# Where the buffers that TensorE reads stand in SBUF: one place in a 2048-byte line instead of two

## The reference

```python
# 1. attention with a state (delta rule): batch 4, 8 heads, 768 steps, head size 48
for t in range(S):
    y[:, :, t] = einsum('bhd,bhde->bhe', q[:, :, t], state)
    v_old = einsum('bhde,bhd->bhe', state, kt)
    state = state + bt * einsum('bhd,bhe->bhde', kt, vt - v_old)
# x = y as 3072 tokens x 384
# 2. eight experts of width 1024; P is a softmax-like gate, balanced in 8 Sinkhorn rounds
out = 0
for e in range(8):
    h = maximum(x @ w1[e], 0)            # 384 -> 1024
    out += P[:, e:e + 1] * (h @ w2[e])   # 1024 -> 384
# 3. one wide layer of width 2048
h = x @ w_in                             # 384 -> 2048
return (h * cos(h)) @ w_out              # 2048 -> 384
```

## Time and profile before

| | |
|---|---|
| median of three executions | 2347.82 us |
| the profiled execution | 2351.72 us |
| its span, first to last instruction | 2350.0 us |
| mean granted TensorE clock | 0.972 of 2.4 GHz |
| TensorE matmul busy | 2256.2 us (96%) |
| VectorE, ScalarE, GpSimd busy | 1012.5, 741.9, 686.6 us |

### The profile page before, as it was taken

The page is one execution under the profiler, slowest core; times in us unless marked ns, Lnnn a source line. Parts: engine busy times, 40 slices in busy tenths (PEclk is TensorE's granted clock), DMA queues, the critical chain, the costliest instruction groups (busy, mean ns, idle before and its releaser), DMA issues.

```text
span 2350.0 us, 40688 instructions
## 1 busy us (share of the span) xinstructions
PE 2256.2 (96%) x15460; PEld 1845.5 (79%) x15460; DVE 1012.5 (43%) x1621; ACT 741.9 (32%) x1288; POOL 686.6 (29%) x504
## 2 busy tenths in 40 slices
PE   3699998999999999999999999999999999999998
PEld 2688886788888888888888888888888877778786
DVE  4876742543232223232323223222323246777676
ACT  5555643311111111111111111111111226666665
POOL 3100001003523333232323232333323244444433
PEclk6689999999999999999999999999999999999999
DMA  5243332202101110111111011111111100000001
GB/s 157 71 116 96 88 95 79 94 14 65 40 27 32 27 45 27 31 27 31 29 43 30 28 31 27 34 37 31 27 31 27 45 22 14 14 14 14 0 14 67
DMA packets 85221, 102.35 MB, mean 44 GB/s; under 512 B 8384, under 2 KB 70144, under 8 KB 85120
## 3 DMA queue, kind: packets, MB, share of 16 engines
q1 hardware_dynamic: 85120, 100.91, 15.5%
HBM read 87.40 MB, written 8.75 MB: 41 GB/s over the span
## 4 chain that ended last, share of the span: by engine, by line
PE 75%; issue 12%; POOL 6%; DVE 4%; ACT 2%; SPq 1%; POOLq 0%; DMA 0%; DVEq 0%; ACTq 0%
PE h L595 5%; PE h L596 5%; PE p_h L595 5%; PE h L597 5%; PE p_h L597 5%; PE p_h L596 5%; POOL hlo L1102 4%; PE am_y L626 4%; PE am_y L624 4%; PE am_y L625 4%; PE chain_y L624 2%; PE chain_y L625 2%; PE chain_y L626 2%; PE o_y L624 2%; PE o_y L625 2%
## 5 line engine op out<-in xcount | busy, mean ns | idle before, releaser
L1081 POOL TENSOR_TENSOR acc<-acc,py 128x512 f32 (+1 forms) x252 | 325.3, 1319 | 760.8 <-DVE py L1385 760.8
L945 ACT ACTIVATE hhi<-h 128x512 fp32r<-128x512 f32 x182 | 109.1, 599 | 790.4 <-PE h L597 790.4
L1352 DVE SCALAR_TENSOR_TENSOR hlo<-h,hhi 128x512 fp32r<-128x512 f32 x182 | 125.9, 692 | 483.9 <-ACT hhi L945 483.9
L1352 DVE SCALAR_TENSOR_TENSOR hlo<-p_h,hhi 128x512 fp32r<-128x512 f32 x182 | 125.9, 692 | 411.7 <-ACT hhi L945 411.7
L1049 POOL TENSOR_TENSOR wlo<-stage,whi (+1 forms) x114 | 156.8, 1377 | 448.7 <-ACT whi L835 423.1
L595 PE MATMUL h<-xhi,whi 128*128 (+1 forms) x690 | 271.1, 393 | 2.4 <-DVE scr L1453 2.4
L596 PE MATMUL h<-xlo,whi 128*128 (+1 forms) x690 | 270.0, 391 | 0.0
L595 PE MATMUL p_h<-xhi,whi 128*128 (+1 forms) x690 | 269.9, 391 | 0.0
L597 PE MATMUL h<-xhi,wlo 128*128 (+1 forms) x690 | 268.7, 389 | 0.0
L597 PE MATMUL p_h<-xhi,wlo 128*128 (+1 forms) x690 | 268.5, 389 | 0.0
L596 PE MATMUL p_h<-xlo,whi 128*128 (+1 forms) x690 | 268.5, 389 | 0.0
(11 more groups left out here) (223 smaller groups left out, 4109.7 us busy)
## 6 DMA issues: line engine op xcount, KB each, us to landing
stage<-wcat SPq DMA_DIRECT2D x40, 768.0 KB, 4.3
pb<-p_scratch SPq DMA_DIRECT2D x84, 256.0 KB, 4.7
kq<-kqt SPq DMA_DIRECT2D x48, 192.0 KB, 3.4
kn<-krow SPq DMA_DIRECT2D x6, 768.0 KB, 5.5
kT<-kta SPq DMA_DIRECT2D x24, 192.0 KB, 5.3
v<-vrow SPq DMA_DIRECT2D x24, 192.0 KB, 3.9
kb<-krow SPq DMA_DIRECT2D x24, 192.0 KB, 4.9
out<-acc SPq DMA_DIRECT2D x6, 768.0 KB, 3.8
```

What stands on the lines that cost most here:

```text
L945: act.activation(hhi[:, j, :], hps[j % 2][:, 0:TILE], ACT.Relu).then_inc(s["hhi_done"], 1)
L1081: pool.tensor_tensor(y, y, py[:, d, :], ALU.add).then_inc(s["added"], 1)
L1352: dve.scalar_tensor_tensor(out=hlo[:, j, :], in0=hps[j % 2][:, 0:TILE], scalar=0.0, in1=hhi[:, j, :].bitcast(F32), op0=ALU.max, op1=ALU.su ...
```

## The change

The eight small buffers move from between `hlo` and `whi0` to the end, behind `py`. Everything between moves down by 1312 bytes. The number, the order, the operands and the waits of the instructions are the same on every engine; only addresses differ.

```diff
     hhi = place("hhi", [P, CH, TILE], F32R)
     hlo = place("hlo", [P, CH, TILE], F32R)
-    wgs = place("wgs", [P, DC, N_EXP])
-    wgr = place("wgr", [P, DC, 2, N_EXP], F32R)
-    prob = place("prob", [P, NB, N_EXP])
-    pm = place("pm", [P, 4])
-    rs = place("rs", [P, NB])
-    cs = place("cs", [P, 2, N_EXP])
-    halfpi = place("halfpi", [P, 1])
-    ident8 = place("ident8", [P, N_EXP])
 
     whi0 = place("whi0", [P, WCOL], F32R)
...
     py = place("py", [P, DC, TILE])
+    small_at = at[0]
+
+    wgs = place("wgs", [P, DC, N_EXP])
+    wgr = place("wgr", [P, DC, 2, N_EXP], F32R)
+    prob = place("prob", [P, NB, N_EXP])
+    pm = place("pm", [P, 4])
+    rs = place("rs", [P, NB])
+    cs = place("cs", [P, 2, N_EXP])
+    halfpi = place("halfpi", [P, 1])
+    ident8 = place("ident8", [P, N_EXP])
     assert at[0] <= nc.sbuf_usable_end
...
-    assert r[0] <= at[0]
+    assert r[0] <= small_at
```

## The result

The changed kernel takes 2313.48 us (median of four executions, 2311.99 to 2314.49); the kernel before, now with four executions, 2345.59 (2342.82 to 2349.22). The ratio is 0.9862 with a 95% interval of 0.9844 to 0.9879: 1.4% faster, 32 us. The forecast was 2316.5 us, 31.5 us less.

What follows compares the result with a forecast made beforehand. TensorE's back-to-back matmuls were taken as the bound. Terms of 25.5 (experts), 5.5 (wide layer) and 0.5 us (early tiles) summed to 31.5 off the median 2347.8: 2316.5 us, own range 2310 to 2325, overall range 2309 to 2352.

Steps and rivals of the forecast that it cites:

- The bound: Some 1,900 of 2,350 us are matmuls in a row on TensorE: their number times the distance between two starts.
- The cause: Downs: stream and next weights' load, at unlike places modulo 512 (or 64, 128, 256), hinder each other by 16 cycles.
- the gate's 0.231: Early gate: 0.231 us a matmul, weights at 224, moving operand at 1440; taken as evidence for distance, expected to stay slow.
- the slower rival: All ups and downs: the moving operand's place alone counts, 128 is slow; ups go to 0.2333, time 2371 us; chance 0.14.
- Term (a): Experts: 91 tiles, each 16.32 us instead of 16.60, gain 25.5 us.
- Term (b): Wide layer: 6.7 us at most, 1.2 given back at 12 pair heads waiting for `hlo`; net 5.5 us.
- Term (c): Early tiles beside the attention: faster downs gain 0.5 us, between 0 and 1.2.
- Term (d): Attention: 768 small matmuls of `stage` with moved buffers change distance; taken as 0, +-3 us.
- Term (e): GpSimd: changed distances could move `hlo`'s time, 2.2 us better or worse at 12 pair heads; taken as 0.
- No change: Whole kernel: distance does nothing, downs slow for another reason such as rewriting of `hhi` and `hlo`; 2348 us, chance 0.24.
- Half done: Whole kernel: only the settled rate improves or other engines hinder TensorE's reads; half the gain left, 2332 us; chance 0.06.

Runs made afterwards that it cites:

- mirror image: Changed kernel with `hhi`, `hlo` and all weights at 128, `xhi` and `xlo` alone at 1440: 2354.96 us, ratio to before 1.0051.
- the pads: Changed kernel, pads ahead of `whi0`, `xhi`, `whi1`: mixed sizes 2362.2, 2349.18, 2361.66 us; 256 ahead of the first two 2312.71; 128 ahead of all three 2359.12.
- short-load runs: Two of three down matmuls of chunks 0 to 2 in the experts load 32 weight columns: 2326.82 us on the changed kernel, 2340.41 on the kernel before.

## Why the prediction was right

*The bound.* TensorE's rate, not its waits: confirmed by the window and by the sections' sums.

*The cause.* The forecast took "unlike places modulo 512 (or 64, 128 or 256)". The mirror image and the run with everything at 1440 show that it is the distance; the pads show that it is modulo 256, with 192 a case in between that depends on its surroundings. My choice among the readings had rested on the gate's 0.231, and the gate, whose weights stay at 224, stayed slow as foretold: 345.17 to 346.56 is 1.39 us for 6.

```profile
345.17 0.40 PE L459 MATMUL o_y<-xhi,wgr 128*8 128x512 f32 x1
...
346.56 0.40 PE L459 MATMUL o_y<-xhi,wgr 128*8 128x512 f32 x1
```

The short-load runs show, though, that a stream with short loads in it is uneven at the good distance too. The gate was thus weaker evidence than I made of it. Without it, the distance and the place of the moving operand fit the rows of before equally well, and choosing right between them was in part luck. Whether its 0.231 comes from the distance or from its 8 columns no run here tells, so the slower rival was more open than I wrote.

*Term (a), experts:* 25.5 us foretold, 25.2 measured; the tile's 16.32 us is exact.

*Term (b), wide layer:* 5.5 foretold, 5.4 measured, but the agreement is luck. The sum took 12 x 0.56 = 6.7 us and gave 1.2 back as 0.1 us of cover lost at the head of each pair. The pair came to 33.10 and not 33.17: the six pairs behind the third gained 0.55 each and lost next to nothing. The 1.2 us went in the first three pairs, which gained 0.50 instead of 1.7. There TensorE stands still several times while the first tiles come through, and behind each stop it starts unevenly; which of these costs it no run separates. TensorE's wait for `hlo`, foretold to grow, fell from 5.2 to 4.5 us.

*Term (c), early tiles:* the settled early downs went to 0.2267 too, but 0.5 us can't be read out of an attention that varies by more.

*Term (d), attention's small products:* no loss seen, and a gain cannot be told from the chance of single executions.

*Term (e), GpSimd:* I allowed that equal places change its `hlo`, and its mean did rise, from 1479 ns to 1516. But not by the places: it is 1516 or 1517 ns in every kernel with the wide layer's matmuls at the good distance, with everything at 128, everything at 1440, or `scr` 512 bytes further, and 1477 to 1494 in all others, among them the two with one operand in three off (1482 and 1485), where `scr` also stands a multiple of 512 bytes from `hhi`. So it goes with the speed of TensorE. VectorE's second step on `scr` went from 1171 to 1122 ns at the same time; that the two shift against each other is my reading and not shown. TensorE's waits show no net cost of it.

*The sum:* the time forecast was 2316.5 us (2347.8 less 31.5 is 2316.3), measured are 2313.48. The medians differ by 32.1 us; in the profiled executions the experts and the wide layer give 30.6. The rest, and the 3 us to the forecast, is no more than the end of the attention varies by. One reading of the rows was loose: two of the slices from the fourth on are below nine tenths, not one, and nothing hangs on it.

*The Trainium skill's rule* ("SBUF — State Buffer", section Who interferes with whom), that TensorE's read ports are independent and it waits for nobody, would have made all these kernels equal, and does not hold here: the same matmuls take 97.92 or 100.80 us a pass by addresses alone.

*The rivals.* No change fell with the result, and with it its reason, since `hhi` and `hlo` are still rewritten all the time. The slower case fell with the result too, since all stream from 128 at 0.2267, and again with the mirror image, where ups stream slowly from 1440. Half done would have needed 2332 us.

## What to carry to other kernels

Where TensorE is busy throughout, read the distance between two starts group by group before the durations, which hold the overlap with the neighbours; groups of equal shape with unequal distances point at addresses. Place every buffer that TensorE reads, moving operands and weights, high and low parts, at the same place modulo 256 bytes, and pad small buffers or put them last. Do it for all: with one operand in three 32 bytes off, the kernel was slower (2363.6 us) than in the unplanned layout (2349.6 beside it).

## What I had not expected

- A single misplaced operand in three costs as much as all three at 233.3 ns would (432 x 0.2333 = 100.8 us): 100.80 us a pass, as against 100.38 with every distance at 128 and 99.60 in the kernel before, whose ups are well placed.
- The rate has a memory. After a disturbed group a well-placed one shows one to eight uneven distances until the starts are 226.7 ns apart, in the order 234, 229, 231, 231, 236, 228, 232, 231, 227 behind nine misplaced ups. A group of nine well-placed downs there averages 231.0 ns, and most of the gain is lost.
- Loads of 32 columns instead of 128 (108 ns instead of 188) made well-placed matmuls slower, 0.2298 instead of 0.2267.
- With all distances right the 432 matmuls of most passes run without a single irregular start: 97.92 us is 432 x 0.22667, which is 544 cycles of 2.4 GHz each. The passes of 97.95 us hold one short irregular stretch.
